# Attention, then a mixture of experts: the last 64 queries of two heads as one block of 128 rows in plain fp32, the spread inverses in the heads' bank

## What is computed

```python
def _attn_ref(q, k, v, w1, b1, w2):          # B, H, S, D = 4, 8, 576, 64
    scores = scale * np.matmul(q, k.transpose(0, 1, 3, 2))
    ...
    scores = scores + bias.transpose(2, 0, 1)[None, :, :, :]     # a small network of the positions
    scores = scores - np.max(scores, axis=-1, keepdims=True)
    attn = np.exp(scores)
    attn = attn / (np.sum(attn, axis=-1, keepdims=True) + 1e-09)
    return np.matmul(attn, v).astype(np.float32)
def _moe_ref(x, w_gate, w1, w2):             # N, D, E, F = 2304, 512, 8, 1024
    P = np.exp(x @ w_gate - max)             # then 8 rounds of balancing over rows and columns
    for e in range(E):
        out += P[:, e:e + 1] * (np.maximum(x @ w1[e], 0.0) @ w2[e])
```

## Time and profile before

| | us |
|---|---|
| median of 3 runs | 1831.27 |
| lowest and highest | 1830.96, 1833.93 |
| the profiled execution | 1830.92 |
| its span, first to last instruction | 1829.1 |
| PE busy in the span | 1817.4 |
| DVE, POOL, ACT busy | 1053.7, 1029.0, 821.8 |

### The profile page before, as it was taken

The page is one execution under the profiler, slowest core; times in us unless marked ns, Lnnn a source line. Parts: engine busy times, 40 slices in busy tenths (PEclk is TensorE's granted clock), DMA queues, the critical chain, the costliest instruction groups (busy, mean ns, idle before and its releaser), DMA issues.

```text
span 1829.1 us, 27894 instructions
## 1 busy us (share of the span) xinstructions
PE 1817.4 (99%) x10222; PEld 1592.9 (87%) x10222; DVE 1053.7 (58%) x1785; ACT 821.8 (45%) x1416; POOL 1029.0 (56%) x721
## 2 busy tenths in 40 slices
PE   8999999999999999999999999999999999999999
PEld 4687788898999999999999999999999999999998
DVE  9877778677555455456545553555455545554553
ACT  8887778534333333343333333333333333333331
POOL 0232345677666666557676666666666666656661
DMA  7754552111111211112211111112221111111110
GB/s 240 237 151 116 132 136 61 47 70 69 70 70 70 70 70 69 70 70 96 77 62 62 65 67 70 70 69 70 70 104 70 70 70 69 70 70 70 70 46 35
DMA packets 44127, 152.47 MB, mean 83 GB/s; under 512 B 9456, under 2 KB 18032, under 8 KB 29680
## 3 DMA queue, kind: packets, MB, share of 16 engines
q1 hardware_dynamic: 43872, 150.90, 25.5%
q10 hardware_dynamic: 144, 0.09, 0.0%
HBM read 135.63 MB, written 15.34 MB: 83 GB/s over the span
## 4 chain that ended last, share of the span: by engine, by line
PE 97%; POOL 1%; DVE 1%; DMA 1%; issue 0%; ACT 0%; SPq 0%; ACTq 0%; DVEq 0%
PE banks L687 14%; PE banks L688 14%; PE banks L686 14%; PE banks L654 13%; PE banks L658 13%; PE banks L656 13%; PE banks L584 4%; PE banks L545 3%; PE banks L527 2%; PE banks L528 2%; PE banks L486 2%; PE banks L555 1%; PE banks L598 0%; POOL total L1369 0%; DMA bias_scratch<-bias_out 0%
## 5 line engine op out<-in xcount | busy, mean ns | idle before, releaser
L1350 POOL TENSOR_TENSOR w_lo<-stage,w_hi 128x1024 fp32r<-128x1024 f32 (+1 forms) x288 | 647.2, 2262 | 530.3 <-ACT w_hi L886 526.8
L1229 DVE TENSOR_TENSOR u<-p_copy,banks 128x384 f32<-128x384 f32 x192 | 106.4, 554 | 628.5 <-PE banks L658 628.5
L688 PE MATMUL banks<-w_hi,h_lo 128*128 128x512 f32 x1152 | 450.2, 391 | 0.0
L687 PE MATMUL banks<-w_lo,h_hi 128*128 128x512 f32 x1152 | 450.0, 391 | 0.0
L686 PE MATMUL banks<-w_hi,h_hi 128*128 128x512 f32 x1152 | 449.1, 390 | 0.0
L1235 DVE SCALAR_TENSOR_TENSOR h_lo<-corner,h_hi 128x384 fp32r<-128x384 f32 x384 | 412.2, 1102 | 0.0
L933 ACT ACTIVATE h_hi<-corner 128x384 fp32r<-128x384 f32 x384 | 196.5, 526 | 271.5 <-DVE corner L1229 268.3
L654 PE MATMUL banks<-x_hi,w_hi 128*128 128x384 f32 x896 | 301.0, 336 | 0.1
L658 PE MATMUL banks<-x_hi,w_lo 128*128 128x384 f32 x896 | 300.3, 335 | 0.0
L886 ACT ACTIVATE w_hi<-stage 128x1024 fp32r<-128x1024 f32 (+1 forms) x288 | 271.5, 974 | 9.1 <-POOL stage L1344 9.1
L922 ACT ACTIVATE p_copy<-banks 128x384 f32<-128x384 f32 x96 | 47.2, 492 | 490.2 <-PE banks L658 490.2
(11 more groups left out here) (136 smaller groups left out, 2458.8 us busy)
## 6 DMA issues: line engine op xcount, KB each, us to landing
stage<-in_expert_w SPq DMA_DIRECT2D x96, 1024.0 KB, 4.8
raw<-in_qk SPq DMA_DIRECT2D x32, 576.0 KB, 7.1
bias_scratch<-bias_out SPq DMA_DIRECT2D x36, 288.0 KB, 2.7
bias<-bias_scratch SPq DMA_DIRECT2D x16, 288.0 KB, 3.0
v_main<-in_v SPq DMA_DIRECT2D x16, 256.0 KB, 2.7
bias<-bias_scratch SPq DMA_DIRECT2D x16, 256.0 KB, 3.7
out<-total SPq DMA_DIRECT2D x4, 768.0 KB, 3.9
out<-total SPq DMA_DIRECT2D x6, 256.0 KB, 2.0
```

The lines of the kernel that those rows point to most:

```text
L687: pe.matmul(dst, h_hi[:, g % 2, f, tokens], lo[:, f], start=False, stop=False)
L688: mm = pe.matmul(dst, h_lo[:, g % 2, f, tokens], hi[:, f], start=False, stop=fp == FPAIRS - 1 and f == 1)
L1229: dve.tensor_tensor(out, other, bank, op).then_inc(combined, 1)
L1350: pool.tensor_tensor(lo, of, hi.bitcast(F32), ALU.subtract).then_inc(w_split, 1)
```

## The change

- The scores of the last block of queries are made for both heads as one block: head 0's 64 rows on partitions 0 to 63, head 1's on 64 to 127. The operands are plain fp32 (`last_q`, `last_k`), loaded for each batch by a new `load_last` on SP; `last_k` lies where the odd head's bias of this block lay. Four matmuls replace eight. There is one reading and one exponential for the block instead of two, nine a batch instead of ten (`READINGS`), and the pairs of score banks alternate by the number of the reading.
- The turn of this block has four transposes of 128 rows and two small matmuls with the identity, one of each head.
- The bias of this block is loaded for both heads to one block of 128 partitions.
- `inv_wide` has nine columns of blocks; its last is spread by two small matmuls. The spread inverses go to bank 6. Their waits become `heads_kept` and, for the next batch's `values`, `scaled`; L555 waits for neither.
- In the tail, product 1 stands after step 2 and product 2 after step 3.

```diff
-TAIL_PRODUCTS = {(0, 0): 0, (0, 1): 3}
+TAIL_PRODUCTS = {(0, 0): 0, (0, 1): 2, (0, 2): 3}
...
+            def load_last(hp, b):
+
+                sp.dma_start(last_q[:], last_qk[hp, b][:, 0:REST]).then_inc(last_in, 16)
+                sp.dma_start(last_k, last_qk[hp, b][:, REST:REST + S]).then_inc(last_in, 16)
...
                     load_pair(0, 1)
                     load_values(0, 0)
+                    load_last(0, 0)
...
-                        sp.wait_ge(biased, 2 * (QC * n + 4) + 1)
+                        sp.wait_ge(biased, READINGS * (n + 1))
                         load_values(*((hp, b + 1) if b < B - 1 else (hp + 1, 0)))
+                        load_last(*((hp, b + 1) if b < B - 1 else (hp + 1, 0)))
...
+            def last_scores(hp, s):
+
+                n, _ = batch(hp, s)
+                pe.wait_ge(last_in, 32 * (n + 1))
+                pe.wait_ge(biased, reading(hp, s, 0) - 1)
+                pe.nop(nofuse=True)
+                for a in range(2):
+                    cols = slice(HALF * a, HALF * a + HALF)
+                    for h in range(2):
+                        rows = head_rows(h)
+                        mm = pe.matmul(banks[rows, score_bank(s, 0) + a, 0:HALF], last_q[rows, :], last_k[rows, cols],
+                                       start=True, stop=True)
+                mm.then_inc(scores_ready, 1)
...
+                    for i in range(KC if qc < KC else KC // 2):
+                        begin = main(h) + i * P if qc < KC else (h * KC // 2 + i) * P
+                        mm = pe.transpose(banks[:, 4 + h, i * P:i * P + P], probs[:, s % 2, begin:begin + P], ident[:])
                     mm.then_inc(turned[h], 1)
                 if exists(hp, s - 1):
                     pe.wait_ge(kept_t[2], at)
-                if rest_read is not None:
-                    pe.wait_ge(*rest_read)
-                if rows < P:
+                if qc < KC:
+                    mm = pe.transpose(rest_bank[:, 0:P], probs[:, s % 2, KC * P:KC * P + BOTH], ident[:])
+                else:
                     pe.nop(nofuse=True)
-                pe.transpose(rest_bank[:, 0:rows], probs[0:rows, s % 2, KC * P:KC * P + 2 * REST],
-                             ident[0:rows, 0:rows]).then_inc(turned[2], 1)
+                    for h in range(2):
+                        rows = head_rows(h)
+                        mm = pe.matmul(rest_bank[rows, 0:REST], probs[rows, s % 2, KC * P:S], ident[rows, rows],
+                                       start=True, stop=True)
+                mm.then_inc(turned[2], 1)
...
                         if exists(hp, s - 1):
-                            pe.wait_ge(heads_kept, 2 * n)
+                            pe.wait_ge(scaled, PIECES * n)
...
-                pe.wait_ge(kept_t[2], hp * STEPS + s + (7 if exists(hp, s + 6 + piece) else 5) +
-                           (piece if exists(hp, s + 6 + piece) else 0))
+                pe.wait_ge(heads_kept, 2 * n + 2)
                 pe.wait_ge(inv_widened, n + 1)
```

More of the change, by code:

```diff
@@ L83, in main, with reading, bass_attention_moe @@
     return 0 if h == 0 else S + REST
-def bass_attention_moe(nc, qk, v, bias_w, gate_w, expert_w, log_table, identity, out):
+def reading(hp, s, h):
+    batches, qc = divmod(s, QC)
+    return hp * READINGS * B + READINGS * batches + 2 * qc + (h if qc < KC else 0)
+def bass_attention_moe(nc, qk, last_qk, v, bias_w, gate_w, expert_w, log_table, identity, out):
     with ExitStack() as ctx:
@@ L529, in scores, with turn @@
                     mm.then_inc(scores_ready, 1)
-            def turn(hp, s, rest_read):
+            def turn(hp, s):
                 n, _ = batch(hp, s)
                 at, qc = hp * STEPS + s, s % QC
-                rows = queries(qc)
                 if not exists(hp, s - 1):
@@ L595, in spread_inverses @@
                 begin, end = PIECE_AT[piece:piece + 2]
-                for qc in range(begin // P, -(-end // P)):
-                    at = INV_AT + qc * P - begin
-                    mm = pe.transpose(rest_bank[:, at:at + P], inv_wide[:, P * qc:P * qc + P], ident[:])
+                if end == S:
+                    pe.nop(nofuse=True)
+                    at = KC * P - begin
+                    for h in range(2):
+                        rows = head_rows(h)
+                        pe.matmul(inverse_bank[rows, at:at + REST], inv_wide[rows, KC * P:KC * P + D], ident[rows, rows],
+                                  start=True, stop=True)
+                for qc in range(begin // P, end // P):
+                    at = qc * P - begin
+                    mm = pe.transpose(inverse_bank[:, at:at + P], inv_wide[:, P * qc:P * qc + P], ident[:])
                 mm.then_inc(spread, 1)
-                return scaled, PIECES * n + piece + 1
             def step(hp, s):
@@ L815, in exponentials @@
                 def exponentials(h):
-                    if not exists(hp, s):
+                    if not exists(hp, s) or s % QC == KC and h == 1:
                         return
                     slot = batch(hp, s)[1]
-                    rows = queries(s % QC)
-                    act.wait_ge(biased, 2 * (hp * STEPS + s) + h + 1)
-                    row = probs[0:rows, s % 2, S * h:S * h + S]
+                    act.wait_ge(biased, reading(hp, s, h) + 1)
+                    row = probs[:, s % 2, S * h:S * h + S]
                     total_at = 2 * (s % QC) + h
-                    act.activation(row, row, ACT.Exp, bias=neg_max[0:rows, 2 * (s % 2) + h:2 * (s % 2) + h + 1],
+                    act.activation(row, row, ACT.Exp, bias=neg_max[:, 2 * (s % 2) + h:2 * (s % 2) + h + 1],
                                    scale=-1.0,
-                                   accum_out=row_sum[0:rows, slot, total_at:total_at + 1]).then_inc(exped, 1)
+                                   accum_out=row_sum[:, slot, total_at:total_at + 1]).then_inc(exped, 1)
                 def keep_turned():
@@ L1076, in scale_heads @@
                 to = x[:].rearrange("p c n -> p (c n)")[:, bass.ds(n * S + begin, end - begin)]
-                dve.tensor_tensor(to, heads[:, slot, begin:end], rest_bank[:, INV_AT:INV_AT + end - begin],
+                dve.tensor_tensor(to, heads[:, slot, begin:end], inverse_bank[:, 0:end - begin],
                                   ALU.mult).then_inc(scaled, 1)
@@ L1111, in step @@
                 for h in range(2):
-                    if exists(hp, s):
+                    if exists(hp, s) and not (qc == KC and h == 1):
                         if s < QC and h == 0:
-                            dve.wait_ge(bias_in[qc], 48 * (hp + 1))
-                        dve.wait_ge(scores_ready, 2 * at + h + 1)
+                            dve.wait_ge(bias_in[qc], (48 if qc < KC else 32) * (hp + 1))
+                        dve.wait_ge(scores_ready, reading(hp, s, h) + 1)
                         if exists(hp, s - 2):
@@ L1134, in step @@
                     n, slot = batch(hp, s - QC)
-                    dve.wait_ge(exped, 2 * at)
+                    dve.wait_ge(exped, reading(hp, s, 0))
                     if exists(hp, s - 15):
@@ L1428 @@
     qk = np.stack([by_pair(q), keys], axis=0).transpose(1, 2, 5, 0, 3, 4)
+    last = np.concatenate([by_pair(q)[:, :, :, KC * P:], by_pair(k)], axis=3)
+    last = last.transpose(0, 1, 2, 4, 3).reshape(PAIRS, B, 2 * D, REST + S)
     vv = by_pair(v).transpose(0, 1, 3, 2, 4).reshape(PAIRS, B, S, 2 * D)
```

76 lines of the change are left out of this document (46 added, 30 removed).

## The result

The median of 21 runs of the changed kernel is 1835.32 us (1833.30 to 1839.66), of 21 runs of the kernel before 1831.37 us (1830.96 to 1833.93). The ratio is 1.0024, 95% interval 1.0017 to 1.0030: slower by 0.24%, inside the predicted range of 1828 to 1838 and 2.3 us above the 1833 forecast. The runs of the changed kernel spread into two groups: 10 of 21 from 1833.3 to 1834.5 (middle 1834.2), 7 from 1838.5 to 1839.7, and four between, from 1835.3 to 1836.4. The kernel before has no second group. The profiled execution took 1838.86 us (span 1837.1) and belongs to the upper one, which lies outside the predicted range. The prediction did not foresee it.

A forecast was written before the change was run, and what follows sets the result against it. TensorE, busy 99% of the span, was taken as the bound. Attention batches -0.4, start +0.8 and hand-over +1.4 gave +1.8 us on 1830.92, 1832.7; with 0.35 to the median, forecast 1833, range 1828 to 1838.

The forecast's parts named there:

- Rival B': Last block's scores: pairing of the heads slips, five slots instead of four, +0.24 us a batch, 1837 us; chance 0.10.
- rival C: Last block's scores: 64-row passes cheaper than thought, gain at most 0.34 us a batch, 1828 us; chance 0.09.
- The gate: Step 3: PE's transposes wait for ACT's exponential, 0.70 us at the shortest; PE savings before it worth at most 0.2 us a batch.
- Part 1: Scores of the last 64 queries: four two-pass matmuls, heads overlapping, take 1.11 us where 1.08 stood.
- Rival B: Last block's scores and small products: the two heads don't overlap, +1.19 us a batch, 1852 us; chance 0.15.
- Part 2: Second piece of spreading the inverses: two small products and two transposes take 0.50 us, where three transposes took 0.33.
- Parts 1 and 2 together: Last block's scores plus second spread piece: 1.61 us after against 1.41 before, +0.20 us a batch.
- Part 3: Inverses moved to bank 6: PE's waits for DVE shrink, -0.16 us in step 3 and -0.07 in step 4.
- Part 4: Turning the last block: four full transposes and two products take 0.70 us, as nine 64-row transposes did; no change.
- Part 5: Start: extra loads ahead of a bias store delay the start of the attention by 0.5 to 1.0 us, counted +0.8.
- Part 6: Hand-over to the experts: nothing covers the wait for u2 before product 3, +1.4 us, which stays since PE is full afterwards.

The follow-up runs named there:

- e10_bank_filled: Kernel before plus inverses in bank 6, expert weights loaded later, the change's product order, and DVE's factor-5 split and u2 ahead of the second scaling: 1828.70 us, ratio 0.9984.
- e4_pool_after_split: Changed kernel with one wait more: POOL starts splitting the second group's weights only after DVE has split all seven factors; median 1835.21 us.
- e3_sum_ahead: Changed kernel with DVE's first combination u2 moved ahead of the second scaling of the last heads; median 1835.59 us.

## Why the prediction was right or wrong, step by step

**The range and the direction held; the sum did not.** It read +1.8 us, and without the wait near 80 us it should have read +2.5 to +2.8. The median is 2.3 above the forecast: some 1 us of it is the hand-over and the batch, and the rest is that wait, which lifts 7 of the 21 runs by some 4.7 us and leaves four more between the groups. That the median stayed inside 1828 to 1838 is in part luck: the width was there for rivals B' and C, which did not come true, and it took in two costs that the prediction did not know of. By the prediction's own mark, slower from 1834.9 on, 1835.32 is just slower, to which it had given 0.34.

**The gate:** never reached, as said. From the end of the exponential to the end of its transposes it is 0.95 us in the changed kernel (208.26 to 209.21) and 0.86 in e10_bank_filled (202.72 to 203.58), where 0.70 would be the gate.

**Part 1, scores:** right. 1.12 us against 1.11. Rival B is refuted: two heads, in different rows of the array, write one bank and overlap. The Trainium skill, TensorEngine Tiling (Array Packing), Gotcha 1, would forbid it, and the 1.12 us speak against that rule as it stands; the Trainium skill, PSUM: Partial Sum Buffer, "Terms", by which different quadrants of a bank may be accessed at the same time, agrees with them. Rival B' (five slots) and rival C (cheaper passes) fall with the same row.

**Part 2, spread:** right. 0.48 against 0.50.

**Parts 1 and 2 together:** counted at +0.20 a batch, measured +0.10. The term of before was too small, not that of after: 1.08 us for eight score passes was read in a step whose transposes had just waited for DVE. Without that wait (e10_bank_filled) the same passes take 1.20 us (201.19 to 202.39), one of them 0.28 instead of 0.13. So 1.60 stands against 1.53, +0.07.

**Part 3, the bank:** right, and the largest gain: -0.22 a batch alone (mean -0.19), where -0.16 and -0.07 were counted.

**Part 4:** right, 0.70 and 0.70. The sum for a batch was -0.03 and is -0.12 (mean -0.11), -1.2 to -1.4 us over the stage and not -0.4.

**Part 5, the start:** the size is right, 0.8 us at the first exponential and 0.6 to 0.7 at the wait for the store. The prediction looked at no other load of that queue. The 16 DMA engines are full again from 66 to 80 us (97% busy in the changed kernel), where a load with 0.5 us to spare waits behind 2 MB of weights. That is the first step that failed, a term put at nothing: the cover of that load was never looked up. Every kernel in the table that keeps the weights ahead of it has a profile with the wait, the kernel before included (1.24 us). The change made it frequent and long (3.31), and moving the weights away ends it. How the change does that is not shown. It is not the extra bytes ahead of the load, for in the queue they stand behind it, and between the last stores and it the queue moves the same bytes in the same order as before. That the new tensor lies elsewhere in memory, or that all loads go out 0.7 us later, are rivals that no run tested.

**Part 6, the hand-over:** right up to the end of the first pass of product 3. From the end of the last value products that is 3.37 us before (331.51 - 328.14) and 4.78 after (337.34 - 332.56): +1.41, and +1.4 was said. The second step that failed is the sentence behind it, "after it PE is full to the end, so it stays". PE was not full: DVE's chain, started 1.4 us later, ran into POOL's split of weights. In the kernel before that split begins at 332.87, and DVE's last one ends at 332.69 (331.74 + 0.95), so they had missed each other by 0.2 us:

```profile
331.74 0.95 DVE L1149 TENSOR_TENSOR x_lo_rest_r<-x,x_hi 128x768 fp32r<-128x768 f32 x1
...
332.87 4.53 POOL L1350 TENSOR_TENSOR w_lo<-stage,w_hi 128x768 fp32r<-128x768 f32 x2 [20.06 <-ACT w_hi L886]
```

ACT and POOL go by the products, which the change moved forward: POOL's split began 4.73 us after the last value products and now begins after 4.43 (336.99 - 332.56). DVE goes by the spread, which the change moved back: its last split began after 3.60 and now begins after 5.01. So it fell behind POOL's. That cost 1.7 us (e4_pool_after_split). The new order of the products as a whole cost 2.15.

## What to carry to other kernels

When an edit shifts one engine's chain against another's, look up every engine that touches the same memory beside it and not only who waits for whom: a gap of 0.2 us between a DVE and a POOL instruction is cover, as a wait is. And when a change touches a saturated queue, find the load with the least to spare anywhere in it, not only the one behind the edit; a transfer that nobody reads for 200 us has no place ahead of it, and moving it was what ended the second group of runs. A joint block that saves DVE and ACT one reading in ten is worth nothing where PE is the bound: it cost 0.1 us a batch. The bank move beside it was the whole gain.

## What was not expected of the hardware

A DVE subtraction of two SBUF operands beside one of POOL's is held back until POOL's instruction has ended (2.60 against 0.95 us), not slowed in proportion. After idle times of PE of 2.82 and 2.51 us the granted clock fell from its full level to 1.2 GHz for a while (mean 0.83 over 10 us, eight transposes in 1.94 us), and after 2.81 us it held (1.00, 1.07 us). The same is seen in the first stage: from 28 to 32 us the mean is 0.58 in the changed kernel's profile, after 2.99 us of idle time, and 1.00 in e3_sum_ahead's, after 3.27. Of one 1 MB load, the last sixteenth can land some 5 us behind the others.
